# Gates in three parts of time, half rows side by side on TensorE, and slot weights in two halves

## The reference

```python
# 1. attention with gates: B, H, S, D = 4, 8, 768, 40; for every time t:
m_new = maximum(f_gate + m, i_gate); f = exp(f_gate + m - m_new); i = exp(i_gate - m_new)
C = f * C + i * outer(v, k);  n = f * n + i * k
y = sigmoid(o_gate) * (C @ q) / maximum(abs(n @ q), 1)
# x = y as 3072 tokens of 320 columns
# 2. soft mixture: 8 experts of 4 slots, phi 320x32, w1 8x320x1024, w2 8x1024x320
logits = x @ phi
slot_input = softmax(logits, over tokens).T @ x
slot_out[e] = maximum(slot_input[e] @ w1[e], 0) @ w2[e]
x2 = softmax(logits, over slots) @ slot_out
# 3. feed-forward, 3072 tokens, w_in 320x2048, w_out 2048x320
out = maximum(x2 @ w_in, 0) ** 2 @ w_out
```

## Time and profile before

| | us |
|---|---|
| median of 3 runs (391.86 to 392.49) | 392.47 |
| the profiled execution | 392.09 |
| its span, first to last instruction | 390.4 |
| TensorE busy in it | 371.8 (95%) |
| VectorE, ScalarE, GpSimd busy | 236.3, 229.8, 81.9 |

### The profile page before, as it was taken

How to read it: one execution, slowest core, us unless ns; L and a number is a source line. 1 busy time by engine, 2 the same in 40 slices (tenths; PEclk the granted TensorE clock), 3 DMA queues, 4 the chain that set the end, 5 groups by cost and what they waited for, 6 DMA issues and landing times.

```text
span 390.4 us, 9581 instructions
## 1 busy us (share of the span) xinstructions
PE 371.8 (95%) x3504; PEld 314.5 (81%) x3504; DVE 236.3 (61%) x556; ACT 229.8 (59%) x455; POOL 81.9 (21%) x122
## 2 busy tenths in 40 slices
PE   2899999989999999999999999999999999999996
PEld 2687777777677776345699999999999999999996
DVE  8767569558846954420487665565556556556553
ACT  3466667667576753021288666666666666666662
POOL 7276556455554730000000000000000000000000
PEclk9999999999999999999999999999999999999999
DMA  6499797787777769969100010010001001001001
GB/s 184 111 270 296 239 267 249 229 250 238 245 239 224 245 228 312 363 226 387 62 2 1 2 67 2 2 53 14 0 0 67 0 0 67 0 0 69 2 0 67
DMA packets 28392, 51.49 MB, mean 132 GB/s; under 512 B 2852, under 2 KB 19684, under 8 KB 28100
## 3 DMA queue, kind: packets, MB, share of 16 engines
q1 hardware_dynamic: 24884, 40.49, 33.3%
q10 hardware_dynamic: 3472, 10.51, 7.8%
HBM read 46.59 MB, written 4.33 MB: 130 GB/s over the span
## 4 chain that ended last, share of the span: by engine, by line
PE 89%; DVE 4%; ACT 2%; issue 2%; ACTq 1%; DMA 1%; POOL 0%; DVEq 0%
PE heads_banks L1119 7%; PE high_banks L1121 7%; PE high_banks L1120 7%; PE high_banks L1119 7%; PE heads_banks L1120 7%; PE heads_banks L1121 7%; PE low_banks L1107 6%; PE heads_banks L829 6%; PE low_banks L808 5%; PE heads_banks L822 3%; PE high_banks L844 3%; PE low_banks L788 3%; PE low_banks L861 3%; PE low_banks L1042 2%; PE high_banks L852 2%; PE low_banks L879 2%
## 5 line engine op out<-in xcount | busy, mean ns | idle before, releaser
L742 ACT ACTIVATE relu_h<-low_banks 128x512 f32<-128x512 f32 x96 | 57.5, 599 | 60.4 <-PE low_banks L1107 60.0
L1432 DVE CAST sq_hi<-sq_h 128x512 fp32r<-128x512 f32 x96 | 41.0, 427 | 66.7 <-ACT sq_h L747 66.1
L1434 DVE TENSOR_TENSOR sq_lo<-sq_h,sq_hi 128x512 fp32r<-128x512 f32 x96 | 66.5, 693 | 3.3
L747 ACT ACTIVATE sq_h<-relu_h 128x512 f32<-128x512 f32 x96 | 60.7, 632 | 3.1
L1120 PE MATMUL high_banks<-wo_lo,sq_hi 128*128 128x320 f32 x192 | 59.3, 309 | 0.0
L1121 PE MATMUL high_banks<-wo_hi,sq_lo 128*128 128x320 f32 x192 | 59.3, 309 | 0.0
L1119 PE MATMUL high_banks<-wo_hi,sq_hi 128*128 128x320 f32 x192 | 59.3, 309 | 0.0
L1119 PE MATMUL heads_banks<-wo_hi,sq_hi 128*128 128x320 f32 x192 | 59.3, 309 | 0.0
L1120 PE MATMUL heads_banks<-wo_lo,sq_hi 128*128 128x320 f32 x192 | 59.1, 308 | 0.0
L1121 PE MATMUL heads_banks<-wo_hi,sq_lo 128*128 128x320 f32 x192 | 59.0, 307 | 0.0
L1162 DVE TENSOR_TENSOR att_w<-low_banks,att_w 128x512 f32<-128x512 f32 x48 | 30.9, 685 | 31.5 <-PE low_banks L808 30.8
(11 more groups left out here) (181 smaller groups left out, 559.0 us busy)
## 6 DMA issues: line engine op xcount, KB each, us to landing
w_sb<-in_w SPq DMA_DIRECT2D x8, 1280.0 KB, 11.1
w_a<-in_w ACTq DMA_DIRECT2D x16, 512.0 KB, 5.4
kv_in<-in_kv SPq DMA_DIRECT2D x24, 320.0 KB, 4.0
qk_in<-in_qk SPq DMA_DIRECT2D x24, 256.0 KB, 3.3
o_in<-in_o_gate SPq DMA_DIRECT2D x24, 160.0 KB, 4.0
out<-out_sb SPq DMA_DIRECT2D x5, 640.0 KB, 3.2
wo_raw<-in_w_out SPq DMA_DIRECT2D x4, 640.0 KB, 11.5
w_b<-in_w ACTq DMA_DIRECT2D x8, 256.0 KB, 3.8
```

The lines of the kernel that those rows point to most:

```text
L742: act.activation(relu_h[:, slot], bank[slot][:, :], ACT.Relu).then_inc(relu_done, 1)
L747: act.activation(sq_h[:, slot], relu_h[:, slot], ACT.Square).then_inc(sq_done, 1)
L1432: dve.tensor_copy(sq_hi[:, slot], sq_h[:, slot]).then_inc(hi_done, 1)
L1434: dve.tensor_tensor(sq_lo[:, slot], sq_h[:, slot], sq_hi[:, slot].bitcast(F32), ALU.subtract).then_inc(lo_done, 1)
```

## The change

- The gates are computed in three parts of 256 times (`GATE_PARTS`). Parts 0 and 1 go to the rows by DMA each by itself (12 DMAs in place of 6); the third goes to DRAM with the rest and its source rows come back from there (`src_rest`). `decay(0, 0)` waits for part 0 alone. `keyw` is made and turned in two goes, the second within step (0, 1). TensorE's unread products before `decay(0, 0)` are 5, not 9. The tiles for later use are cleared after steps (0, 2) and (0, 3). SP waits for the copies in DRAM before its loop over the steps, now behind the third part.
- The last chunk's logits are computed for two thirds before its x is there, and for the last third after it. In the last round `dispatch_exp` waits for two instructions of the maximum, not four, the transposed logits go to another bank (`last_turn`), and `row_relative` comes after `slotsT`.
- The last 64 rows of `w1` and `w_in` lie as 64 rows for one set and 64 rows for the other, and their products use 64 rows of the array each (`expert_rest`). `slot_twice`, `row_half` and `keep_turned` go. The order of the experts' products is another.
- The slot weights are made, split, spread and copied in two halves of 256 columns, the second beside the first hidden tiles, and the first tile of the feed-forward is squared and split in halves.

```diff
@@ start, SP
+            def direct_rows(part):
+                sp.wait_ge(rows_one_hot, part + 1)
+                sp.wait_ge(gate_act, act_count(A_CUM, part))
+                direct_cum(0, part)
+                sp.wait_ge(gate_vec, vec_count(G_CUMLO, part))
+                direct_cum(1, part)
+                sp.wait_ge(gate_act, act_count(A_SRC, part))
+                direct_src(sp, 0, 0, part)
+                sp.wait_ge(gate_vec, vec_count(G_SRCLO, part))
+                direct_src(sp, 1, 0, part)
+            sp.wait_ge(rows_fixed, 1)
+            direct_rows(0)
             load_kv(0, 1)
             load_o(0, 0)
+            direct_rows(1)
...
+            sp.wait_ge(gate_act, act_count(A_SRC, 2))
+            sp.wait_ge(gate_vec, vec_count(G_SRCLO, 2))
+            sp.dma_start(cum_dram, ...); sp.dma_start(src_dram, ...)
             sp.wait_ge(rows_stored, 32)
+            for r in range(2): ... row_y[..., t0:S] from src_dram, then_inc(src_rest, 16)
@@ start, ACT
+            one_hot(0); cum_high(0); src_high(0)
+            direct_src(act, 0, 1, 0); direct_src(act, 1, 1, 0)
+            one_hot(1); raise_keyw(0, 0, 2 * L)
+            cum_high(1); src_high(1)
+            direct_src(act, 0, 1, 1); direct_src(act, 1, 1, 1)
             copy_v(0, 0)
             decays(0, 0)
@@ act_step
+                if (b, c) == (0, 0):
+                    cum_high(2); src_high(2)
                 if cur:
                     copy_heads(b, c)
                     raise_fade(b, c + 1)
+                    if (b, c) == (0, 0):
+                        raise_keyw(2, 2 * L, S)
@@ start, DVE
+            forget_logs(0); source_logs(0); key_logs(0, 2 * L)
+            forget_logs(1); source_logs(1)
+            forget_logs(2)
+            keep_keyw(1, 0, 2)
             weigh(0, 0)
+            source_logs(2); key_logs(2 * L, S)
@@ start, PE
-            pe.wait_ge(gate_vec, G_CUM)
-            stay_awake(9)
+            stay_awake(5)
             decay(0, 0)
+            turn_keyw(0, 0, 2)
@@ step (0, 2) on POOL: mask(b, c) goes ahead of weigh_keys, which waits for keyw_ready 2
@@ last chunk, PE
-            stay_awake(5)
-            turn_x(B - 1, NC - 1, 1)
-            stay_awake(2)
-            logit(B - 1, NC - 1)
+            logit(B - 1, NC - 1, (0, 1))
+            stay_awake(2)
+            turn_x(B - 1, NC - 1, 1)
+            stay_awake(1)
+            logit(B - 1, NC - 1, (2,))
@@ dispatch_exp, ACT
-                act.wait_ge(max_chain, 4 * rb + 4)
-                act.activation(shrink ...)
+                act.wait_ge(max_chain, 4 * rb + 2)
                 act.activation(disp_e ...)
+                act.wait_ge(max_chain, 4 * rb + 3)
+                act.activation(shrink ...)
@@ turn_disp, PE
-                pe.wait_ge(row_chain, 7 * rb + 2)
+                if rb < B - 1:
+                    pe.wait_ge(row_chain, 7 * rb + 2)
@@ experts, PE
+            def expert_rest(n):
+                for q in range(4):
+                    for g in range(2):
+                        rows = slice(DP * g, DP * (g + 1))
+                        mm = pe.matmul(bank[2 * g + n][QUAD * q:QUAD * (q + 1), :], slotsT[rows, 2],
+                                       w1_b[rows, q, 512 * n:512 * (n + 1)], start=False, stop=True)
+                mm.then_inc(hidden, 2)
             expert_first(0)
-            turn_comb(B - 1, 0)
+            expert_rest(0)
             expert_first(1)
-            turn_comb(B - 1, 1)
             turn_hidden(0, 0)
             turn_hidden(1, 0)
+            turn_comb(B - 1, 0)
+            expert_rest(1)
+            turn_comb(B - 1, 1)
             expert_second(0, 0)
             turn_hidden(0, 1)
             turn_hidden(1, 1)
-            expert_second(0, 1)
             expert_second(1, 0)
-            turn_outs(0)
+            expert_second(0, 1)
             expert_second(1, 1)
+            turn_outs(0)
+            turn_outs(1)
             stay_awake(1, bank[3])
-            turn_outs(1)
-            stay_awake(2, bank[3])
@@ slot weights, PE
+            def slot_weights(h):     # 256 columns; the last 64 rows on row groups 0 and 64
+                for k in range(KC):
+                    for i in range(4) if k < 2 else (0, 2, 1, 3):
+                        ...
+            def spread_weights(h):   # waits for sw_high, sw_low of h; h == 1 also for the copies of h == 0
+            slot_weights(0)
+            slot_weights(1)
+            spread_weights(0)
             pe.wait_ge(sw_ready[0], 1)
             hidden_tile(0, 0)
             hidden_tile(0, 1)
+            spread_weights(1)
+            stay_awake(2, bank[3])
+            for i in range(2):
+                pe.wait_ge(sw_ready[i], 4)
@@ slot weights, DVE
             (wo_hi, wo_lo of the first four tiles, as before)
+            low_weights(0); copy_weights(0, 1); low_weights(1); copy_weights(0, 3)
+            copy_weights(1, 1); copy_weights(1, 3)
@@ first tile, ACT (DVE splits it in halves likewise)
+                act.activation(relu_h[:, 0, 0:256], bank[0][:, 0:256], ACT.Relu)
+                act.activation(sq_h[:, 0, 0:256], relu_h[:, 0, 0:256], ACT.Square)
+                copy_weights(1, 0)
+                copy_weights(1, 2)
+                act.activation(relu_h[:, 0, 256:512], bank[0][:, 256:512], ACT.Relu)
+                act.activation(sq_h[:, 0, 256:512], relu_h[:, 0, 256:512], ACT.Square)
```

More of the change, by code:

```diff
@@ new lines, in src_high, with raise_keyw @@
+            def src_high(part):
+                a, z = GATE_PARTS[part]
+                act.wait_ge(gate_vec, vec_count(G_SRC, part))
+                act.activation(src_parts[:, 0, a:z], src[:, a:z], ACT.Copy).then_inc(gate_act, 1)
+            def raise_keyw(part, a, z):
+                act.wait_ge(gate_vec, vec_count(G_KEYW, part))
+                act.activation(keyw[:, a:z], keyw_log[:, a:z], ACT.Exp).then_inc(gate_act, 1)
+            one_hot(0)
+            cum_high(0)
+            src_high(0)
@@ L868, in step_exps, with logit @@
                 return 2 * (step(b, c) + 3)
-            def logit(b, c):
-                pe.wait_ge(xT_ready, step(b, c) + 1)
+            def logit(b, c, thirds=range(TRI)):
+                pe.wait_ge(xT_ready, step(b, c) - 1 + thirds[-1])
                 pe.wait_ge(phi_loaded, 32)
@@ L964, in pe_step, with turn_keyw @@
                     logit(*before(b, c))
+            def turn_keyw(part, c0, c1):
+                pe.wait_ge(gate_act, act_count(A_KEYW, part))
+                for c in range(c0, c1):
+                    mm = pe.transpose(turn_ps[:, c], keyw[:, L * c:L * (c + 1)], ident[0:NS, 0:NS])
+                mm.then_inc(keyw_turned, 1)
             def stay_awake(count, spare=heads_bank):
@@ L1082, in _ @@
-            pe.wait_ge(win_loaded, 32)
-            for k in range(KC):
-                for i in range(4):
-                    part, cols = (outsT[:, k], win_sb[:, k, 512 * i:512 * (i + 1)]) if k < 2 else \
-                        (outsT[:, 2 + i // 2], win_rest[:, 512 * (i % 2):512 * (i % 2 + 1)])
-                    mm = pe.matmul(bank[3][QUAD * i:QUAD * (i + 1), :], part, cols, start=k == 0, stop=k == KC - 1)
-            mm.then_inc(sw_done, 1)
-            stay_awake(4, bank[0])
-            pe.wait_ge(spread_ready, 2)
@@ new lines, in spread_weights @@
+            def spread_weights(h):
+                pe.wait_ge(sw_high, h + 1)
+                pe.wait_ge(sw_low, h + 1)
+                for i in range(4):
+                    rows = slice(QUAD * i, QUAD * (i + 1))
+                    if h == 1:
+                        pe.wait_ge(sw_ready[i % 2], i // 2 + 1)
+                    for part in range(2):
+                        mm = pe.matmul(bank[4 + i][:, 256 * h:256 * (h + 1)], spread[rows, part].rearrange("p a b s -> p (a b s)"),
+                                       sw_cols[rows, part, 256 * h:256 * (h + 1)], start=part == 0, stop=part == 1)
+                    mm.then_inc(sw_spread, 1)
@@ L1137, in pe_block @@
                         hidden_tile(tb + 1, f + 2 - NF)
-                    if first and f == 0:
-                        stay_awake(5, bank[3])
-                        for i in range(2):
-                            pe.wait_ge(sw_ready[i], 2)
                     if first and (f == 0 or f >= WO_PART):
@@ new lines, in clear_sums, with shape_tiles @@
+            def clear_sums():
+                dve.memset(slot_acc[:, :], 0.0)
+                dve.memset(slot_sum[:, :], 0.0)
+                dve.memset(neg_max[:, :], -LOWEST)
+            def shape_tiles():
+                dve.memset(fold_own[:, :, :], 0.0).then_inc(fold_cleared, 1)
+                dve.wait_ge(consts_in, 16)
+                dve.tensor_reduce(thirds[:, :], ident.rearrange("p (q s) -> p q s", q=4), AX.X, ALU.add)
+                dve.wait_ge(fold_cleared, 1)
+                for e in range(E):
+                    rows, own_slots = slice(QUAD * (e % 4), QUAD * (e % 4 + 1)), slice(SLOTS_PER_E * e, SLOTS_PER_E * (e + 1))
```

(2 more changed lines are left out.)

377 lines of the change are left out of this document (219 added, 158 removed).

## The result

| | before | changed |
|---|---|---|
| median, us | 392.48 (391.86 to 393.58, 4 runs) | 389.23 (385.74 to 390.15, 4 runs) |
| ratio to before, 95% interval | | 0.9901 (0.9874 to 0.9928) |
| the profiled execution, us | 392.09 | 388.81 |
| its span, us | 390.4 | 387.1 |
| first attention product, us | 19.22 | 16.04 |

Steps are counted from 0 in this part; a step's length is the time from its first `attend` product to the next one's. The result lies above the range given (381.0 to 387.0). Four stretches gained (3.18, 1.14, 3.5 and 2.2 us). The 24 steps, for which the prediction's sum held a loss of 0.7, lost 6.3. The long loop, which it left alone, is 0.4 longer: 191.9 us from the second tile's first product to the end, 191.5 before.

The account below looks back on a forecast made before the run. Chains of waits ahead of 198.92 us, at the start and from about 151, were taken to decide everything. Savings of 2.1 + 1.35 + 3.75 + 2.1 = 9.3 gave 382.8, median 383.1 us; range 381 to 387.

Parts of the forecast that it names:

- The range: Whole kernel: 381 to 387 us, from the start's full 2.8 and a smooth hand-over to both smaller rivals together.
- The start's earlier end: Up to the first attention product: exponential at about 13.7 in place of 16.47, product and `attend` 2.8 us earlier.
- I count 0.7 for all this (0 to 1.8): Early attention steps: the part of the start's 2.8 us given back through late handoffs, more transposes and SP's late step 3 loads.
- the start is given back: Rival: SP's late step 3 loads queue later ones, the start keeps about 0.3 of 2.1; 385.4 us, chance 0.18.
- The low clock: Rival at the start: fewer unread products leave TensorE at its low clock, steps cost up to 5.5 us each; chance 0.04.
- Tail: Routing after attention: logits ahead of x, earlier exponential, shorter slot sums and weight loads; 1.35 us saved (0.6 to 1.7).
- Experts: Experts' products: half rows side by side and reordered work filling waits; 3.75 us saved (2.0 to 4.2).
- eight tiles together: Half-row expert products run at once, in about 0.9 us; the rival that they don't: 384.8 us, chance 0.12.
- To the feed-forward: From the experts' end to the second tile's first product: 10.1 us instead of 12.25, 2.1 saved (0.5 to 3.0).
- the wait ahead of the second tile: Feed-forward's start: TensorE done with the first `out_tile` at 190.4, waiting 1.3 us for the second tile.
- a DMA wait at the scores of step 3 over 1 us: Attention step 3: listed as a sign that the prediction was wrong.
- clock below 1.0 after 13: Granted clock after 13 us: listed as a sign that the prediction was wrong.

Follow-up runs that it names:

- Experiment 3: The changed kernel with SP's loads of k, v, q and k for step 3 and gate o for step 2 ahead of its store wait; 384.97 us.
- experiment 8: The kernel before with only the new start, SP's step 3 loads ahead of its wait, gate o behind the stores, ACT's first `w_a` late; 390.29 us.
- experiment 2: The kernel before with only the new start (gates in three parts, fewer unread products, SP's new order), `w_b` in its old form; 393.63 us, ratio 1.0047.
- 1: The changed kernel with the old start taken back (gates in one piece, nine unread products, SP's old load order); 387.06 us, ratio 0.9874.
- 5: Experiment 3 with gate o of step 2 loaded between the stores and their wait, and ACT's first `w_a` load put late; 384.79 us.
- 4: The changed kernel with ACT's two `w_b` issues put behind the tanh and the copy of xT of the same step; 388.35 us, ratio 0.9888.
- 11: Experiment 5 with VectorE's second `key_logs` behind the weighing of step 1 and ScalarE's exponential of them behind its tanh; 385.64 us.
- 14: Experiment 5 with `w_a` at steps 1 to 16 and `w_b` last, one transfer per step at steps 16 to 23; 384.23 us, ratio 0.9810.
- 17: Experiment 5 with the `w_b` transfers of experts e and e + 4, on opposite halves of the partitions, paired in one step; 385.62 us.
- experiment 13: Experiment 5 with `w_b` first, one transfer per step at steps 1 to 8, and `w_a` at steps 8 to 23; 383.72 us, ratio 0.9781.
- 12: Experiment 5 with `w_b` issues spread one per step and the second `key_logs` and its exponential put late; 384.51 us.
- 6: Experiment 5 with `w_b` in four transfers over 128 partitions instead of eight over 64; 403.27 us, ratio 1.0280.
- 7: The changed kernel with the old start and `w_b` in four transfers over 128 partitions; 401.55 us, ratio 1.0220.
- 9: Experiment 5 with the two `w_b` issues of every fifth step spread over that step and the next, one each; 384.94 us.
- 18: The changed kernel with the `w_b` transfers of experts e and e + 4, on opposite halves of the partitions, paired in one step; 388.08 us.

## Why the prediction was wrong

- *The start's earlier end*: right. 3.18 for 2.8, the exponential at 13.32 for 13.7; ScalarE's order set it.
- **The step that failed: "I count 0.7 for all this (0 to 1.8)".** The prediction had the late loads (last part of q at "about 24.4", measured 24.36), had them land at about 28, and took the landing and the scores to meet within 0.5 us. They landed at 30.3. I used a landing of 3.5 us from a queue in its steady state, and it took 5.9: SP issued all that it had held back one behind the other, and in the windows the half idle queues (98 GB/s) became full ones (314). The waits of steps 2 and 3 cost 2.4 us, the third part's own work 1.2 (0.87 and 0.36), 3.6 for the 0.7 counted. Experiment 3 shows that the first goes with the order of the loads, and experiment 8 that the second stays: with SP's loads ahead of the wait and ACT's first `w_a` late, the start keeps 2.0.
- *Its rival* "the start is given back" named the right place and was priced at 1.8 us back. Alone, the new start gives back 2.7 of 3.2 at full clock (experiment 2), and in most executions more than all of it.
- *A term that the sum didn't have*: the half rows of `w_b` were priced on TensorE alone. Their transfers are 0.15 us longer to issue each, on a queue that stands ahead of the tanh, and slow the full queues. This costs 0.3 us at steps 10 and 15 and 0.1 at step 20 wherever both issues stand ahead of the tanh (experiments 1, 3, 5). In two profiled executions (the changed kernel and 1) one of these issues was slow and the low clock came behind it; but the kernel before has a slow issue of the old form too (46.24 us), so the form isn't shown to bring it.
- *The low clock*: the prediction looked for it at the start, for lack of unread products. In the profiled execution the start was at 1.0 from 12 us on, and it came at step 11, after an idle of 1.34 us, for 1.5 us. But what the rival describes came in other executions, at a small price: of the 16 kernels profiled with the new start, five (experiments 4, 5, 11, 14 and 17) have a granted clock of 0.5 for 3.4 us from 16 to 17 us on, and step 0 takes 0.7 us longer. The prediction let the ten unread products run at 0.43 each and end at 12.6, and they did here (8.25 to 12.5). In those five they ran faster, in 2.97 to 3.37 us for 4.29, so that they ended sooner and TensorE idled 0.82 to 1.46 us ahead of the products at 13.95; in the eleven others that idle time is 0.65 or less. The two go together in all sixteen, but no experiment forced it.
- *Tail*: 1.14 for 1.35. *Experts*: 3.5 for 3.75, eight tiles together. *To the feed-forward*: 10.06 for 10.1, in part by luck: the wait ahead of the second tile is 0.35, not 1.3, and the rest of the stretch is about 0.9 longer than counted. The first two stand, with their sizes a little off. *The long loop*, left out of the sum, is 0.4 longer; no experiment looked for the reason.
- *The range* reached to 387, with a sum of small rivals. It left out what the transfers do to each other: the changed kernel's one execution at a mean clock of 0.999 took 385.74 us, inside it, the other three did not.

What would have shown it stood in the list: "a DMA wait at the scores of step 3 over 1 us" and "clock below 1.0 after 13" both came true.

Best version: experiment 13, 383.72 us, 2.2% faster than before, where the change as made is 1.0% faster (12 and 14, at 384.51 and 384.23, are not told apart from it).

## What to carry to other kernels

When a change puts a wait into the engine that issues the loads, list every load behind it, and move those that don't depend on it ahead; a stretch of idle queues is paid back as a stretch of full ones, in which the landing times of the steady state don't hold. When a tile gets another layout for the engine's sake, price its transfer too: how many partitions, what its slowest dimension is, and which queue its longer issue holds up. When unread products bridge a wait, count their end by the fast pace as well as by the slow one: the gap that is left may be what lets the clock fall. And a loss of a few microseconds of this kind comes with a spread between executions: the changed kernel's was 4.4 us, that of experiment 13 1.2. The kernel before isn't free of it: of its 13 executions beside experiments 5 to 8, the three with a mean clock of 0.996 took 393.33 to 394.11 us, the ten others 391.75 to 392.71.

## What the hardware showed that I had not expected

- Slow DMA issues go with instruction loads. Between 13 and 140 us the changed kernel has three issues of over 1 us (60.06, 75.77 and 102.43 us), and single packets of its instruction queue start at 60.01, 75.65 and 102.58. In the kernel before it is five of five. One of them is `w_b` at 46.24, 1.30 us, packet at 46.17. It is the longest piece of the chain of waits from 20 to 148 us, and steps 5 and 6 take 0.36 longer together than in experiment 8:

```profile
46.24 1.30 ACTq L620
```

  The queues of the changed kernel from 75.5 to 77 us (packets, MB, share of 16 engines):

```profile
q8 instruction: 1, 0.02, 4.8%
```

  These packets come at other times in another kernel (73.53 us in the kernel before, 75.65 in the changed one), so an edit elsewhere can move a slow issue onto a bad place of ScalarE's order. Over all the profiles but those of 6 and 7, whose queues stall anyway, 42 of 48 issues of over 1 us between 13 and 140 us have a packet of an instruction queue within 0.4 us, and 14% of the shorter ones. The six without are in 4 (125.67 us), 8 (97.42), 9 (all its three) and 17 (31.55). A packet alone isn't enough either: run 5 has 14 of them in that stretch and no issue over 1 us. It is a coincidence in time and was not forced by an experiment.
- A granted clock of 0.5 came back in mid-attention after single idle times of TensorE of 1.05 to 1.34 us (the changed kernel, experiments 1 and 4), and cost the steps under it 1.3 to 1.6 us each time. Such an idle time doesn't always bring it: 1.65 us in the changed kernel, 1.55 in experiment 2, 1.13 in 4 and 1.48 in 18, all between 28 and 34 us, were followed by a clock of 1.0.
- Products on two row groups and four column groups run together: the 16 over half rows hold TensorE for 1.02 us, changes of shape included; one after the other by row group they would have taken 1.73.
